# Transposes three steps and value products five steps behind the scores, in a fused attention and mixer kernel on one core

## The reference

```python
q, k, v: (2, 8, 768, 64) float32; n_sink = 4, window = 128
scores = q @ k.T / 8
keep = (key < n_sink) | (0 <= query - key < window)
a = softmax(where(keep, scores, -1e9));  x = (a @ v) -> (2, 768, 512)

h = relu(x @ w_in)                        # (2, 768, 1024)
u, v = h[..., :512], h[..., 512:]
v_n = (v - mean(v)) / sqrt(var(v) + 1e-6)
x = (u * (w_spatial @ v_n + b_spatial)) @ w_out

u = x + (relu(x.T @ w_tok1) @ w_tok2).T   # w_tok1 (768, 256)
out = u + relu(u @ w_ch1) @ w_ch2         # w_ch1 (512, 1536)
```

## Time and profile before

| | |
|---|---|
| median of 3 runs | 509.5 us (508.4 to 509.59) |
| the profiled execution | 508.11 us, its span 506.3 us |
| mean granted clock of TensorE | 0.986 |
| PE busy | 495.1 us (98%) |
| DVE, ACT, POOL busy | 211.2, 173.1, 154.9 us |
| loads and stores | 33.55 MB, 67 GB/s in the mean |

### The profile page before, as it was taken

One profiled execution on the slowest core, in us unless ns is written; L12 is line 12 of the kernel. 1 busy time (PEld: TensorE's weight loads), 2 busy tenths in 40 slices (PEclk: granted clock), 3 DMA queues, 4 the chain that ended last, 5 costly groups with the idle time before them and its releaser, 6 DMA issues.

```text
span 506.3 us, 7183 instructions
## 1 busy us (share of the span) xinstructions
PE 495.1 (98%) x2678; PEld 438.1 (87%) x2678; DVE 211.2 (42%) x528; ACT 173.1 (34%) x365; POOL 154.9 (31%) x163
## 2 busy tenths in 40 slices
PE   6899999999999999999999999999999999999997
PEld 4788999999999999999888898888888888888885
DVE  5577876777576317754222242122131131211212
ACT  5677766666665242112432232110010010010010
POOL 3544443533323488602205057970000000000000
PEclk9599999999999999999999999999999999999999
DMA  7454323432221234300202013420020000200002
GB/s 239 151 174 162 105 88 97 141 109 88 81 65 46 65 86 129 88 1 5 74 0 79 6 53 97 141 64 0 1 84 1 0 1 0 74 10 0 1 0 83
DMA packets 19190, 34.04 MB, mean 67 GB/s; under 512 B 2256, under 2 KB 4560, under 8 KB 19152
## 3 DMA queue, kind: packets, MB, share of 16 engines
q1 hardware_dynamic: 19008, 33.55, 21.1%
q10 hardware_dynamic: 144, 0.00, 0.0%
HBM read 30.39 MB, written 3.15 MB: 66 GB/s over the span
## 4 chain that ended last, share of the span: by engine, by line
PE 92%; DMA 2%; POOL 2%; DVE 1%; issue 1%; ACT 1%; SPq 0%; DVEq 0%; ACTq 0%
PE bank L955 24%; PE bank L956 24%; PE bank L957 24%; PE bank L1028 7%; PE bank L994 4%; PE bank L970 2%; PE bank L971 2%; PE bank L1036 2%; PE bank L1010 1%; PE bank L1194 1%; DMA stage<-w_in 1%; DMA stage<-w_sp 1%; POOL wsp_lo L538 1%; DMA par_i<-params 1%; POOL vn_lo L549 1%
## 5 line engine op out<-in xcount | busy, mean ns | idle before, releaser
L944 DVE SCALAR_TENSOR_TENSOR hch_lo<-bank,hch_hi 128x512 fp32r<-128x512 f32 x36 | 24.9, 691 | 153.8 <-ACT hch_hi L732 153.8
L732 ACT ACTIVATE hch_hi<-bank 128x512 fp32r<-128x512 f32 x36 | 21.5, 598 | 169.0 <-PE bank L957 169.0
L613 ACT ACTIVATE probs<-masked,small 128x288 f32<-128x288 f32 (+1 forms) x96 | 48.8, 509 | 39.2 <-DVE small L784 38.5
L957 PE MATMUL bank<-up_hi,wc_lo 128*128 128x512 f32 x144 | 56.0, 389 | 0.0
L956 PE MATMUL bank<-up_lo,wc_hi 128*128 128x512 f32 x144 | 56.0, 389 | 0.0
L955 PE MATMUL bank<-hch_hi,wc_hi 128*128 128x512 f32 x144 | 56.0, 389 | 0.0
L956 PE MATMUL bank<-hch_lo,wc_hi 128*128 128x512 f32 x144 | 56.0, 389 | 0.0
L955 PE MATMUL bank<-up_hi,wc_hi 128*128 128x512 f32 x144 | 56.0, 389 | 0.0
L957 PE MATMUL bank<-hch_hi,wc_lo 128*128 128x512 f32 x144 | 56.0, 389 | 0.0
L784 DVE CUSTOM_DVE_ANT_0 masked<-bank,masks 128x288 f32<-128x288 f32 (+1 forms) x96 | 40.8, 427 | 36.3 <-PE bank L971 32.0
L516 POOL TENSOR_TENSOR k_lo<-k_raw,k_hi 128x512 fp32r<-128x512 f32 x24 | 30.7, 1280 | 72.1 <-ACT k_hi L581 72.1
(11 more groups left out here) (123 smaller groups left out, 1029.1 us busy)
## 6 DMA issues: line engine op xcount, KB each, us to landing
k_raw<-kT SPq DMA_DIRECT2D x24, 256.0 KB, 2.9
q_raw<-qT SPq DMA_DIRECT2D x24, 256.0 KB, 3.0
stage<-w_c SPq DMA_DIRECT2D x24, 256.0 KB, 2.7
v_sl<-vL SPq DMA_DIRECT2D x12, 264.0 KB, 2.8
outT<-out_sb SPq DMA_DIRECT2D x12, 256.0 KB, 2.6
stage<-w_sp SPq DMA_DIRECT2D x12, 192.0 KB, 2.6
stage<-w_in SPq DMA_DIRECT2D x8, 256.0 KB, 3.5
stage<-w_out SPq DMA_DIRECT2D x4, 256.0 KB, 3.0
```

Of the source, the lines that this page charges most:

```text
L613: act.activation(probs[:, n % N_PROB, 0:w], masked[:, n % N_MASKED, 0:w], ACT.Exp, bias=least[:, n % 8:n % 8 + 1], scale=-1.0).then_inc(ex ...
L732: act.activation(hch_hi[:, u[2] % N_HCH, :], bank[:, :], ACT.Relu).then_inc(hi_ready, 1)
L944: dve.scalar_tensor_tensor(out=hch_lo[:, f % N_HCH, :], in0=bank[:, :], scalar=0.0, in1=hch_hi[:, f % N_HCH, :], op0=ALU.max, op1=ALU.subt ...
L957: return pe.matmul(out, a_lo, b_hi, start=False, stop=last, skip_group_check=skip)
```

## The change

The two lags go from 2 and 4 to 3 and 5. So the transposes of a pair, its value products and the transposes of an x tile all move one step later against the scores, the quarters, the masks and the exponentials. With an odd lag, pairs were turned in odd steps; now it is even ones. The quarters stay where they are. The sinks' probabilities are gathered one step earlier (step 4g + 3 instead of 4g + 4).

`q_high(1)` moves ahead of ACT's loop and `q_low(1)` to DVE's step 1 (it was 2). The keeps for later masks go from DVE's step 1 to 3, the first mask by ACT from step 2 to 4, the flag from DVE's step 2 to 5. SP issues the loads of queries and keys of group 3, two weight pieces and the sinks' values ahead of its wait for the flag instead of behind it.

DVE's general path becomes one loop over 96 tiles, whose offset it counts up in memory; its body stands in the program once, not six times. None of it runs with these inputs.

```diff
-TURN_LAG = 2
-VALUE_LAG = 4
+TURN_LAG = 3
+VALUE_LAG = 5
...
-                for g in range(2, N_GROUP + 4):
-                    if 3 <= g < N_GROUP:
+                for g in range(3, N_GROUP + 4):
+                    if 4 <= g < N_GROUP:
                         load_qk(g)
...
-                    if 3 <= g + 1 < EARLY:
+                    if 5 <= g + 1 < EARLY:
                         stage_in(g + 1)
-                    if g == 3:
-                        load_sink_values(0)
...
             load_v(1)
+            load_qk(3)
+            stage_in(3)
+            load_sink_values(0)
+            stage_in(4)
...
             k_high(1)
+            q_high(1)
             for n in range(N_STEP + 4):
...
-                if n == 2:
+                if n == 4:
                     mask_by_act((MASK_SECOND, second_keep, P), (MASK_SECOND + P + SINKS, diag_keep, P))
...
-                if n % 4 == 0 and n // 4 - 1 in sink_n:
-                    sinks_gather(n // 4 - 1)
+                if n % 4 == 3 and n // 4 in sink_n:
+                    sinks_gather(n // 4)
...
-                if n % 4 == 1 and n // 4 + 1 < N_GROUP:
+                if n % 4 == 1 and 2 <= n // 4 + 1 < N_GROUP:
                     q_high(n // 4 + 1)
...
-            def general_head(g):
-                for i in range(NT):
-                    n = [0]
-                    at_ = g * (NT * G_X) + i * G_X
...
+            def general_tile(t):
...
+                then(dve.tensor_scalar(tile_at, tile_at, float(P), None, ALU.add))
...
-                        with dve.Fori(0, HEADS) as g:
-                            general_head(g)
+                        dve.memset(tile_at, 0.0).then_inc(g_zero, 1)
+                        dve.memset(minus_at, 0.0).then_inc(g_zero, 1)
+                        dve.wait_ge(g_zero, 2)
+                        with dve.Fori(0, HEADS * NT) as t:
+                            general_tile(t)
...
-                if n % 4 == 2 and n // 4 + 1 < N_GROUP:
+                if n == 1:
+                    q_low(1)
+                if n % 4 == 2 and 2 <= n // 4 + 1 < N_GROUP:
                     q_low(n // 4 + 1)
-                if n == 1:
+                if n == 3:
                     later_keeps()
-                if n == 2:
+                if n == 5:
                     general_flag()
```

More of the change, by code:

```diff
@@ L253, in build @@
         g_x = at("g_x", C_VN + S * 10, [D])
-        g_small = at("g_small", C_VN + S * 10 + D, [4])
+        g_small = at("g_small", C_VN + S * 10 + D, [6])
+        tile_at, minus_at = g_small[:, 4:5], g_small[:, 5:6]
         xg = nc.dram_tensor("xg", [HEADS, NT, P, D], F32).ap()
@@ L828, in normalise @@
                                   ALU.subtract, ALU.mult).then_inc(normed, 1)
-            def general_head(g):
-                for i in range(NT):
-                    n = [0]
-                    at_ = g * (NT * G_X) + i * G_X
[L835 to L856, removed]
-                    then(dve.tensor_scalar(g_small[:, 1:2], first_bank[0][:, D:D + 1], EPS_SUM, None, ALU.add))
-                    then(dve.reciprocal(g_small[:, 2:3], g_small[:, 1:2]))
-                    assert n[0] == G_SUM
-                    dve.wait_ge(g_stored, g * (16 * NT) + 16 * i + 16)
-                    then(dve.tensor_scalar(g_x[:, :], first_bank[0][:, 0:D], g_small[:, 2:3], None, ALU.mult))
-                    then(dve.tensor_copy(g_small[:, 3:4], g_small[:, 2:3]))
-                    assert n[0] == G_X
@@ new lines, in general_tile, with then @@
+            def general_tile(t):
+                n = [0]
+                def then(ins):
+                    n[0] += 1
+                    ins.then_inc(g_step, 1)
+                    dve.wait_ge(g_step, t * G_X + n[0])
+                then(dve.tensor_scalar(g_keep, g_rel, tile_at, par[:, 1:2], ALU.add, ALU.is_lt))
+                then(dve.scalar_tensor_tensor(out=g_keep, in0=g_rel, scalar=minus_at, in1=g_keep, op0=ALU.is_ge, op1=ALU.mult))
+                then(dve.scalar_tensor_tensor(out=g_keep, in0=g_key, scalar=par[:, 0:1], in1=g_keep,
+                                              op0=ALU.is_lt, op1=ALU.max))
+                then(dve.tensor_scalar(g_hole, g_keep, -MASKED, MASKED, ALU.mult, ALU.add))
+                dve.wait_ge(g_scored, t + 1)
+                for c in range(2):
+                    cols = slice(HALF * c, HALF * c + HALF)
+                    then(dve.scalar_tensor_tensor(out=g_masked[:, cols], in0=first_bank[c][:, 0:HALF],
+                                                  scalar=-float(D) ** -0.5, in1=g_keep[:, cols],
+                                                  op0=ALU.mult, op1=ALU.mult))
+                then(dve.tensor_tensor(g_masked, g_masked, g_hole, ALU.add))
+                then(dve.tensor_reduce(g_small[:, 0:1], g_masked, mybir.AxisListType.X, ALU.min))
+                assert n[0] == G_LEAST
+                then(dve.tensor_scalar(tile_at, tile_at, float(P), None, ALU.add))
+                then(dve.scalar_tensor_tensor(out=tile_at, in0=tile_at, scalar=float(S), in1=tile_at,
+                                              op0=ALU.is_lt, op1=ALU.mult))
+                then(dve.tensor_scalar(minus_at, tile_at, -1.0, None, ALU.mult))
+                dve.wait_ge(g_valued, t + 1)
+                then(dve.tensor_scalar(g_small[:, 1:2], first_bank[0][:, D:D + 1], EPS_SUM, None, ALU.add))
+                then(dve.reciprocal(g_small[:, 2:3], g_small[:, 1:2]))
+                dve.wait_ge(g_stored, t * 16 + 16)
+                then(dve.tensor_scalar(g_x[:, :], first_bank[0][:, 0:D], g_small[:, 2:3], None, ALU.mult))
+                then(dve.tensor_copy(g_small[:, 3:4], g_small[:, 2:3]))
+                assert n[0] == G_X
```

3 lines of the change are left out of this document (2 added, 1 removed).

## The result

| | median (range), us | runs |
|---|---|---|
| before | 508.95 (508.19 to 509.59) | 4 |
| changed | 515.42 (514.28 to 516.18) | 4 |

The ratio is 1.0121, with an interval of 1.0101 to 1.0141: 6.5 us slower. The forecast was 511.7 with a range up to 514.2, so the direction was right and the size too small by a factor of three (+2.2 forecast). The profiled execution took 515.76 us with a span of 514.0, against 508.11 and 506.3.

What follows compares the result with a forecast made beforehand. PE was taken to bound the kernel, busy 495.1 of 506.3 us. Start -2.0, gather -0.4, x tiles +4.2 and sink keys +0.4 sum to +2.2 us, giving 511.7 from the median of 509.5, range 508.6 to 514.2.

Steps and rivals of the forecast that it cites:

- the start: First 30 us up to v0: queries earlier, shorter DVE branch, clock perhaps back sooner; 2.0 us gained, far ends 0 and 6.0.
- x tiles: PE's matmuls behind each x tile's transposes: x turned later, its low part late, PE waits; +4.2 us, lower end 2.
- sink keys: Second batch's sink keys, score 56: load queued behind a value load, so PE waits; +0.4 us (none to 0.5).
- gather: Sinks' probabilities gathered one step earlier: removes a sink transpose's listed 0.2 us wait and perhaps smaller gaps; -0.4 us (0.2 to 0.8).
- the queries: Query splits: group 1 earlier was said not to pass on; no cost was put for q_low behind 30 us.
- the first matmul behind each wait: On PE after each x wait: runs unpipelined, 0.1 us each, 0.8 together, left to the upper end.
- the branch: DVE's branch near 15.41 us: skipping about 40 instructions, not 165, cuts 3.43 us to 0.1 to 0.4.
- rival D: X tiles: low part ready sooner because ACT and DVE stand idle, so the 4.2 us go; 507.5 us, chance 0.10.
- Rival B: First 30 us: gains twice as much, 4 us, as the clock hardly falls or returns early; 509.7 us, chance 0.20.
- Rival C: DVE's branch stays slow for a reason other than length, only new waits come; 513.2, or 514 with unpipelined matmuls; chance 0.17.

Runs made afterwards that it cites:

- e15: The changed kernel run and profiled once more, nothing altered; 514.54 us, ratio 1.0119.
- e1: The kernel before with only the two lags at 3 and 5; 519.67 us, ratio 1.0195.
- e2: The changed kernel with the lags back at 2 and 4, all else kept; 506.14 us, ratio 0.9930.
- e5: The changed kernel with the quarters of the first mixer product one step later too; 509.47 us, ratio 1.0016.
- e4: The kernel before with only DVE's general path as a loop, so its branch skips less; 506.39 us, ratio 0.9936.
- e9: The changed kernel with only the second batch's sink keys loaded two places sooner in SP's list; 514.92 us, ratio 1.0112.
- e14: The kernel before with the general path as a loop and the sinks' gather one step sooner, lags 2 and 4; 505.82 us, ratio 0.9934.
- e6: The changed kernel with q_low put ahead of the odd pair's copy in DVE's step; 520.72 us, ratio 1.0233.
- e10: The changed kernel with the queries split one step sooner, q_high on ACT and q_low on DVE; 522.45 us, ratio 1.0260.
- e3: The changed kernel with each x tile transposed one step sooner, lags 3 and 5 for the rest; 533.92 us, ratio 1.0493.
- e8: The kernel before with only the transposes of x two steps later; 540.58 us, ratio 1.0615.

## Why the direction was right and the size wrong

The terms fall into two parts, the start up to v0 and what lies behind it. Behind v0 the forecast was 4.2 (x tiles) + 0.4 (sink keys) - 0.4 (gather) = +4.2 us, and the profiles show +8.05 and, in e15, +7.6. This is where the prediction failed: the x tiles were put at 4.2 and cost 5.6, the queries were put at nothing and cost 1.0, the sink keys were put at 0.4 and cost 0.6 to 1.0, and some 0.8 us more stand in no wait that I can name.

- **The x tiles, forecast +4.2.** The mechanism is shown (e1, e2 and e5 agree), with the tiles, the places and the latency as forecast. The size is 5.6 by the trace and 6.0 by e5's time. Of the 1.4 more, 0.9 is the first matmul behind each wait, 0.11 each; I had put it at 0.1 each, outside the sum in the upper end. It belongs in, since a wait without it doesn't exist. The other 0.5 is at tiles 4 and 9, where q_low ran beside POOL's vn_lo and delayed the mask and x_lo (below).
- **The start, forecast -2.0.** v0 starts 0.4 and 1.8 us sooner in two profiles of the changed kernel, against one of before. The medians, less what the stretch behind v0 shows, give 6.5 - 8.05 = -1.6 and, in e15's group, 5.4 - 7.6 = -2.2; this is an estimate, as it puts the stretch of one profile under the median of several runs. So the term was near right, in part by luck: the branch did fall, as forecast, but e4 shows that it alone is worth 3.15 us at lags 2 and 4, more than I had put for the whole start. At lags 3 and 5 part of that seems to be taken back (v0 at 29.59 and 28.20, against 28.22 in e2); with the spread of the clock, which I hadn't named, two profiles don't settle it.
- **The sink keys, forecast +0.4.** The score waited 0.9, 1.0 by the distance of the starts (0.4 and 0.6 in e15, at 95.5 us). The wait is real and e9 removes it, worth 0.9 and 0.4 by the stretch. I had the distance right to 0.6 us, which here was more than the term.
- **The gather, forecast -0.4:** right, -0.4 by the stretch (e14 against e4, e2 against before).
- **Missing: the queries.** A term for q_low behind 30 us stood nowhere; I even counted its new place for rival D. Three scores behind 30 us wait for it, by the distances of the starts 0.3, 0.4 and 0.3 us, 1.0 in all; e2 has no such wait. That it is late because the pairs changed from odd to even steps, so that it now stands behind a pair's copy, is argued only: e6 and e10, made to undo it, moved other waits and tell nothing of it. Here is tile 4's, where it hits x as well:

```profile
78.84 1.28 POOL L553 TENSOR_TENSOR vn_lo<-v_sb,vn_hi 128x512 fp32r<-128x512 f32 x1
79.12 1.54 DVE L778 SCALAR_TENSOR_TENSOR q_st<-q_raw,q_st 64x512 fp32r<-64x512 f32 x1
...
80.69 0.46 DVE L789 CUSTOM_DVE_ANT_0 masked<-bank,masks 128x288 f32<-128x288 f32 x1
80.71 0.33 PE L981 MATMUL bank<-k_hi,q_st 128*128 128x128 f32 x1
...
81.07 0.69 DVE L816 TENSOR_TENSOR x_lo<-bank,x_hi 128x512 fp32r<-128x512 f32 x1
```

The sum behind v0 by the first profile: 5.6 + 1.0 (keys) + 1.0 (queries) - 0.4 (gather) = +7.2, of the 8.05 measured. The missing 0.8 stands in no listed wait; it is spread over the distances of many matmuls, whose order the lags change, and its cause is open. With the start, -1.6 or -2.2, the 6.5 and 5.4 us of the medians come out because the start was taken from them, so that is no check of it.

Rival B was wrong, since the start didn't gain 4. D was wrong in its mechanism: x_lo was not ready sooner, and the waits came. Rival C had the right neighbourhood in time, 514, for the wrong reason: the branch did become fast. The rule of the Trainium skill, page "Runtime: NRT & Kernel Launch", section "Instruction fetch mechanics", that a taken branch to a far target pays for a fetch, agrees with e4. That page's figure of 512 instructions doesn't explain it by itself, since the old path skipped about 165. No run shows where the old target lay, so why some 165 were already too many stays open.

## What to carry to other kernels

Where two hand-written schedules share an engine, shift both or none: a lag that moves a producer against its consumer by one step costs (latency - the work left between + 0.11 us here) each time it comes out above zero, and moving the consumer along gave it back (e5). Before an item is moved, ask what else stands in its new step on each engine and which banks it shares; e3, e6 and e10 each moved a wait and enlarged it. And test the parts of a bundle apart: here a path that never runs was worth 3 us, hidden under a lag that cost 9. Where the start varies from one execution to the next, compare a stretch behind it that holds the same work: it told 0.4 us apart (e14) where the times could not.

## What the runs showed of the hardware

- A split of 64 x 512 on DVE with both inputs in SBUF took 0.69 us alone. In the changed kernel it met a running POOL instruction with two inputs in SBUF five times behind 10 us; it then took 1.28 to 1.69 us and ended each time 0.54 to 0.55 us after POOL. DVE's instructions with one input in PSUM kept their time in the same place, x_lo and the pair's copy 0.69. In e10, POOL ran from 67.26 to 68.54, and q_low ended at 69.10, 0.56 later. So DVE seems to have stood still until POOL was done, then run. The Trainium skill, page "SBUF — State Buffer", section "Terms", says that DVE and GpSimd share a port pair by an exclusive lock, held for the full instruction, and that the loser blocks: the trace agrees, with 1.54 us from 79.12 beside POOL's 1.28 from 78.84.
- DVE's branch over some 165 instructions took 3.43 us, 3.9 in e1 and 4.0 in e8. With about 40 to skip, the next instruction came 0.5 us behind it in the changed kernel and in all twelve other kernels that have the loop.
- Waits of 0.3 to 0.8 us for x_lo left the clock at 2.4 GHz in every case, and so did the waits of up to 1.4 us in e3 and 1.7 us in e6; in e8 waits of 1.8 to 2.0 us, and one of 1.5, were followed by 3.4 us at 1.2 GHz in six of twelve cases.
- The length of the half-clock stretch in the first 28 us differed between executions of one program, 13.7 and 10.2 us, and v0 started 1.4 us apart.
